# A new head, natural logits by transposes, increments behind the gathering, and an early softmax of c, in a fused attention and expert kernel

## Chip, cores, metric

The kernel runs on one core of one Trainium2 chip. The metric is the device time of one execution in microseconds (us), the median of three runs. The engines are TensorE (PE, with its weight loads as PEld), VectorE (DVE), ScalarE (ACT), GpSimd (POOL) and SyncE (SP), which here only issues DMAs.

## The reference

```python
# 1: linear attention with decay; batch 4, 8 heads, 768 steps, head size 48
for t in range(S):
    cur = einsum('bhd,bhe->bhde', u[None] * kt, vt)
    y[:, :, t] = einsum('bhd,bhde->bhe', rt, state + cur)
    state = wt[:, :, :, None] * state + einsum('bhd,bhe->bhde', kt, vt)
# 2: gated MLP on x = y as 3072 x 384; w_in 384 x 2048, w_out 2048 x 384
h = x @ w_in;  x = (h * clip(h + 3, 0, 6) / 6) @ w_out
# 3: soft mixture of 8 experts with 4 slots each, hidden size 1024
logits = x @ phi                                   # 3072 x 32
d = softmax of logits over the tokens;  slot_input = d.T @ x
slot_out[e] = max(slot_input[e] @ w1[e], 0) @ w2[e]
c = softmax of logits over the slots;   out = c @ slot_out
```

## The kernel before

The 3072 tokens are 24 tiles ("units") of 128, in six groups of four: tile n is sequence part n // 4 of batch n % 4. Every engine has its program written out by hand, and semaphores order them.

**Head.** `for n in range(B)` treats the first four tiles. TensorE does for each: `score` (8 heads as pairs in two row halves, 16 passes, L421), `turn_keys` (L430), `diagonal` of the next tile (8 passes of 2 columns, L458), `attend_first` (16 passes of 48 columns, L471), `increment` (L446), `turn_x` (L500) and one `stay_warm` (a 512-column matmul of no use but to keep the engine working, L532). VectorE scans the decays of the next tile (`scan_suffix` L773, `restart_prefix` L778, `scan_prefix` L785), masks the scores (`mask_first` L809), finishes y (L818), multiplies r by its decays (L794) and takes the low half of x (`low_x`, L833). GpSimd multiplies keys by decays (`decay_keys`, L1256) and r by k (`multiply_rows`, L1234), ScalarE copies out of PSUM. SP's queue sends the rows of four tiles, half of w_in, the rows of tile 4, w_outT, and, as buffers come free, the rows of tile 5 and the other half of w_in.

**Steps.** Then a loop over s runs 96 steps (16 per group of four tiles). Step s makes one block of 128 hidden units for the 512 tokens of group s // 16: `mlp(s)`, nine matmuls of 512 columns (three K-tiles, each as high*high, high*low, low*high in 16-bit halves, L514 to L516), into one of two PSUM banks; ScalarE makes the relu (L1123), VectorE gates (L860) and transposes (`turn_gated`, L870). mlp(s) waits for the gate of s - 2. Between them stands attention for the coming group's tiles, one tile per four steps by phase: score in phase 0, mask (L799) and scan in 1, keys, increment in 2, `attend` (L483 to L493) and prefix scan in 3. `low_scores` on GpSimd (L1247) makes the low half of the scores after ScalarE's high half (L1082).

**w_in's halves.** The weights are split into 16-bit halves in eight pieces: `high_w` on ScalarE (L1111), `low_w` on VectorE (L850), piece s // 2 + 1 in each even step of group 0.

**Group ends.** phi is folded into w_out beforehand (`weigh_phi`, L524). `add_logits` (L544) sums logits in four row blocks; ScalarE copies them to `l_part`, `fold_logits` (L551) sums the blocks. In step 2 of the next group VectorE finds the maximum, ScalarE makes alpha (the rescaling of earlier groups) and then `weight` = exp (L1138); VectorE transposes it (L892). `natural_logits` (L556) makes logits with tokens in rows, in step 2; ScalarE copies them (`copy_logits`, L1142). In step 3 follow the increment and `gather_slots`, 64 small matmuls in four banks (L570), which VectorE adds to `acc` in step 4.

**Tail.** After the last gathering the banks are copied out (L1193 on ScalarE, L1030 on VectorE), folded with the inverse sum, transposed, multiplied by w_out, and given to the experts: `apply_w1` (L686), transposes, `apply_w2` (L711), `pick_slots` (L720), the final matmuls (L754) and 12 stores. The softmax of c over all 24 tiles is made in the same stretch (VectorE L1025 to L1046, ScalarE L1190 and L1198), and `turn_c` (L704), three times eight transposes of c, stands between the expert matmuls.

## Time and profile before

| | |
|---|---|
| runs | 452.33, 452.84, 454.29 us; median 452.84 |
| profiled execution | 455.68 us; its span, from the first to the last instruction, 454.0 |
| mean granted TensorE clock | 0.946 |
| busy share of the span | PE 94%, PEld 52%, DVE 75%, ACT 33%, POOL 40% |
| DMA | 69.35 MB, 153 GB/s over the span |

"x16" behind a row says that it stands for sixteen instructions. A row's duration of a matmul holds the time in which it overlaps the next one, so what a pass costs is read from the distance of two starts. The granted clock is the share of TensorE's full clock: 1.00 is 2.4 GHz, 0.50 is 1.2 GHz.

### The profile page before, as it was taken

Reading aid. Unit: us, or ns where it says so; the run is one execution under the profiler, and the core shown is the slowest. Engines: PE = TensorE matmul, PEld = TensorE weight load, DVE = VectorE, ACT = ScalarE, POOL = GpSimd, SP = SyncE. Lnnn points to the kernel's source line nnn. Section 1 sums busy time; section 2 is a strip of 40 time slices with the busy share of each in tenths; the row PEclk is TensorE's granted clock in tenths of the full one; section 3 lists DMA queues with packets and bytes.
Section 4 is the critical chain, followed back from the end, with each engine's and each line's share of the span. In section 5 each row is a group of like instructions: output and inputs, shape, how many; then the busy total and the mean of one; then the engine's idle time right before and its main releaser. Section 6 shows DMA issues by size and latency. Waiting matters only on the chain.

```text
span 454.0 us, 9636 instructions
## 1 busy us (share of the span) xinstructions
PE 427.3 (94%) x3891; PEld 238.2 (52%) x3891; DVE 340.9 (75%) x539; ACT 148.4 (33%) x250; POOL 180.1 (40%) x174
## 2 busy tenths in 40 slices
PE   7999997888999999999999999998999999999982
PEld 3898654444555555556555555464554534433420
DVE  7555589989998989888898998889776676472233
ACT  1221323542433334414344144342432323212122
POOL 5614255575544565446556435654370000000000
PEclk9555699999999999999999999999999999999987
DMA  8996130341933222340343213330005963469919
GB/s 215 300 381 223 61 115 1 115 113 64 337 107 114 77 70 83 115 116 11 104 116 113 86 31 114 114 114 18 37 2 206 423 222 124 181 250 423 395 62 359
DMA packets 15245, 69.35 MB, mean 153 GB/s; under 512 B 2016, under 2 KB 2656, under 8 KB 13152
## 3 DMA queue, kind: packets, MB, share of 16 engines
q1 hardware_dynamic: 15200, 68.73, 43.7%
q8 instruction: 31, 0.51, 0.4%
q14 instruction: 14, 0.11, 0.1%
HBM read 64.00 MB, written 4.72 MB: 151 GB/s over the span
## 4 chain that ended last, share of the span: by engine, by line
issue 39%; PE 33%; POOL 19%; DVE 4%; DMA 1%; ACT 1%; POOLq 0%; SPq 0%; DVEq 0%
POOL att L1256 5%; PE hid L514 4%; PE hid L516 4%; PE hid L515 4%; POOL att L1228 4%; POOL att L1226 3%; POOL att L1241 3%; POOL att L1274 3%; PE hid L711 2%; PE l_ps L570 2%; PE l_ps L544 2%; PE y_ps L471 2%; PE sc_ps L421 1%; PE hid L686 1%; PE sc_ps L686 1%
## 5 line engine op out<-in xcount | busy, mean ns | idle before, releaser
L1123 ACT ACTIVATE relu<-hid,three 128x512 f32<-128x512 f32 x96 | 65.9, 687 | 149.6 <-PE hid L516 149.0
L514 PE MATMUL hid<-x_split,w_split 128*128 128x512 f16 x288 | 109.9, 381 | 3.5 <-DVE gated L860 3.5
L515 PE MATMUL hid<-x_split,w_split 128*128 128x512 f16 x288 | 109.6, 380 | 0.0
L516 PE MATMUL hid<-x_split,w_split 128*128 128x512 f16 x288 | 109.4, 380 | 0.0
L860 DVE SCALAR_TENSOR_TENSOR gated<-relu,hid 128x512 f32<-128x512 f32 x96 | 65.2, 680 | 29.6 <-ACT relu L1123 29.0
L870 DVE STREAM_TRANSPOSE ring<-gated 128x512 f32<-128x512 f32 x96 | 68.3, 711 | 3.3
L1247 POOL TENSOR_TENSOR att<-att 128x1024 f16<-128x1024 f32 x20 | 39.9, 1996 | 64.6 <-ACT att L1082 64.6
L1265 POOL TENSOR_TENSOR att<-att 112x512 f32<-112x512 f32 x19 | 24.3, 1280 | 68.7 <-DVE att L785 68.7
L514 PEld LDWEIGHTS hid<-x_split,w_split 128*128 128x128 f16 x288 | 28.3, 98 | 40.8 <-issue 9.6
L516 PEld LDWEIGHTS hid<-x_split,w_split 128*128 128x128 f16 x288 | 28.2, 98 | 34.4 <-issue 0.5
L515 PEld LDWEIGHTS hid<-x_split,w_split 128*128 128x128 f16 x288 | 28.2, 98 | 25.2 <-issue 0.6
L1256 POOL TENSOR_TENSOR att<-att 112x512 f32<-112x512 f32 x22 | 29.6, 1343 | 14.4 <-DVE att L773 10.3
L421 PEld LDWEIGHTS sc_ps<-att 48*128 48x128 f32 x384 | 26.7, 210 | 16.2 <-issue 14.5
L421 PE MATMUL sc_ps<-att 48*128 48x128 f32 x384 | 31.6, 309 | 3.3 <-issue 2.1
L483 PE MATMUL y_ps<-att 112*128 112x96 f32 x160 | 33.7, 295 | 0.6 <-DVE att L844 0.3
L818 DVE SCALAR_TENSOR_TENSOR att<-y_ps,att 128x384 f32<-128x384 f32 x24 | 13.2, 549 | 24.2 <-PE y_ps L471 13.2
L773 DVE TENSOR_TENSOR_SCAN att<-att 112x517 f32<-112x517 f32 x22 | 28.0, 1272 | 1.3 <-POOL att L1256 1.1
L785 DVE TENSOR_TENSOR_SCAN att<-att 112x517 f32<-112x517 f32 x22 | 27.8, 1265 | 0.1
L483 PEld LDWEIGHTS y_ps<-att 112*128 112x128 f32 x160 | 25.0, 189 | 5.6 <-issue 3.7
L570 PE MATMUL l_ps<-ring,soft 32*32 32x512 f32 x192 | 25.5, 594 | 2.0 <-DVE soft L892 2.0
L570 PE MATMUL sc_ps<-ring,soft 32*32 32x512 f32 x384 | 26.1, 598 | 0.0
L1105 ACT ACTIVATE x_split<-y_ps 128x384 f16<-128x384 f32 x24 | 11.8, 490 | 43.2 <-PE y_ps L500 42.7
(202 smaller groups left out, 768.7 us busy)
## 6 DMA issues: line engine op xcount, KB each, us to landing
att<-nat_dram SPq DMA_DIRECT2D x20, 576.0 KB, 4.2
att<-rkT_dram SPq DMA_DIRECT2D x22, 448.0 KB, 5.6
att<-w_dram SPq DMA_DIRECT2D x5, 1536.0 KB, 14.1
att<-wT_dram SPq DMA_DIRECT2D x22, 226.2 KB, 4.7
out_dram<-w_split SPq DMA_DIRECT2D x12, 384.0 KB, 3.9
stage<-w_in_dram SPq DMA_DIRECT2D x2, 1536.0 KB, 13.7
ring<-w_outT_dram SPq DMA_DIRECT2D x1, 3072.0 KB, 17.2
stage<-w_dram SPq DMA_DIRECT2D x2, 1536.0 KB, 9.2
```

The lines of the kernel that those rows point to most:

```text
L421: last = pe.matmul(sc_bank[j][:, cols], k_dec[n % 2][rows, cols], r_dec[n % 2][rows, cols], start=True, stop=True)
L483: pe.matmul(both, r_dec[n % 2][0:PD, p * P:(p + 1) * P], state[b][0:PD, p, :], start=True, stop=False, skip_group_check=True)
L514: pe.matmul(hid[s % 2][:], high, x_high, start=(q == 0), stop=False)
L515: pe.matmul(hid[s % 2][:], high, x_low, start=False, stop=False)
L516: last = pe.matmul(hid[s % 2][:], low, x_high, start=False, stop=(q == KT - 1))
L570: ins = pe.matmul(dg_bank[a][SLOTS * c:SLOTS * (c + 1), :], weight_T[SLOTS * a:SLOTS * (a + 1), b * SLOTS:(b + 1) * SLOTS], ring_group(g, ...
L773: nc.vector.tensor_tensor_scan(suffix[0:PD, ::-1], w_rows_of(n)[0:PD, ::-1], mark[0:PD, ::-1], 1.0, ALU.mult, ALU.add).then_inc(suffix_don ...
L860: nc.vector.scalar_tensor_tensor(gated_tile(s), relu_tile(s), 6.0 * GATE, hid[s % 2][:], ALU.min, ALU.mult).then_inc(gated_done, 1)
L870: nc.vector.transpose(ring_tile(s), gated_tile(s)).then_inc(gated_turned, 1)
L1123: nc.scalar.activation(relu_tile(s), hid[s % 2][:], ACT.Relu, bias=three[:], scale=GATE / H_SCALE)\
L1247: nc.gpsimd.tensor_tensor(scores_lo, scores, scores_hi, ALU.subtract).then_inc(scores_lo_done, 1)
L1256: nc.gpsimd.tensor_tensor(dst, keys, decay, ALU.mult).then_inc(k_dec_done, 1)
```

## The change

In the head the idle matmuls are cut in three parts that wait for the scans, and two more stand ahead of each `attend_first` and one behind the diagonal; the diagonal's matmuls write their two columns 48 times, attend_first computes two heads' columns at once (the second is overwritten by its own matmul); the diagonal goes behind attend_first, the increment behind turn_x; GpSimd clears the state first; the fold matrix is made by ScalarE. Around step 0 the increment of tile 4, the third weigh_phi and sum_diag move back, the gates of steps 0 and 1 and the scan of tile 5 forward. Low halves 2 to 7 of w_in are made by GpSimd, from pieces that ScalarE scales first. At group ends the weight is made ahead of alpha; the first 32 rows of the folded logits are copied to SBUF, and natural_logits becomes transposes of these, just ahead of gather_slots (behind it in the last group), with the increment behind it. The softmax of c for 20 of 24 tiles is made in the last group (GpSimd, VectorE, ScalarE), in place; turn_c(0) and (1) go ahead of the last gathering; the first pick_slots goes behind the last apply_w2, and half of w2[4] is loaded earlier, into x_late. Buffers that stood there move. The core of the diff:

```diff
-        def split_at(s):
-            return s // 2 + 1 if s % 2 == 0 and s // 2 + 1 < W_PIECES else None
+        def scaled_behind(s):
+            return {0: 3, 4: 4, 5: 5, 8: 6, 9: 7}.get(s)
+
+        def split_behind(s):
+            return {1: 2, 2: 3, 5: 4, 6: 5, 9: 6, 10: 7}.get(s)
...
                 load_nat(n)
-            sp.wait_ge(w_lo_done, W_PIECES)
+            sp.wait_ge(w_lo_done, 2)
+            sp.wait_ge(w_lo_rest_done, W_PIECES - 2)
             for e in range(2):
...
                 sp.dma_start(w1_place[e], w1[e]).then_inc(w1_in[1], 16)
+            sp.dma_start(x_late, w2[4][:, 0:UNIT // 2]).then_inc(w2_late_in[0], 16)
             sp.wait_ge(l_ready, STEPS)
...
                 cols = slice(half * UNIT // 2, (half + 1) * UNIT // 2)
-                for e in (4, 6, 7):
+                for e in (6, 7) if half == 0 else (4, 6, 7):
                     sp.dma_start(w2_place[e][:, cols], w2[e][:, cols]).then_inc(w2_late_in[half], 16)
...
                 for p in range(PB):
-                    last = pe.matmul(hid[1][:, 2 * p:2 * p + 2], rk_prod[n % 2][0:PD, p * P:(p + 1) * P],
-                                     u_rows[0:PD, 2 * p:2 * p + 2], start=True, stop=True, skip_group_check=True)
+                    last = pe.matmul(hid[1][:, p * 2 * D:(p + 1) * 2 * D].rearrange("p (o j) -> p o j", j=2),
+                                     rk_prod[n % 2][0:PD, p * P:(p + 1) * P],
+                                     u_rows[0:PD, 2 * p:2 * p + 2].rearrange("p (o j) -> p o j", o=1)
+                                     .broadcast_to([PD, D, 2]), start=True, stop=True, skip_group_check=True)
                 last.then_inc(diag_ready, 1)
...
                     for j in range(2):
-                        cols = slice((2 * p + j) * D, (2 * p + j + 1) * D)
+                        h = 2 * p + j
+                        cols = slice(h * D, min(h + 2, H) * D)
                         last = pe.matmul(y_ps[:, cols], scores[:, (j * PB + p) * P:(j * PB + p + 1) * P],
...
             def natural_logits(g, n):
+                pe.wait_ge(l_copied, g + 1)
                 pe.wait_ge(state_added, min(n, LAST_INC) - B)
                 for t in range(B):
-                    last = pe.matmul(inc_ps[:, DM + t * SLOTS:DM + (t + 1) * SLOTS], l_part[:, t * P:(t + 1) * P],
-                                     fold32, start=True, stop=True, skip_group_check=True)
+                    last = pe.transpose(inc_ps[:, DM + t * SLOTS:DM + (t + 1) * SLOTS],
+                                        l_part[0:SLOTS, t * P:(t + 1) * P], ident[0:SLOTS, 0:SLOTS])
                 last.then_inc(nat_logits_ready, 1)
...
                 pe.wait_ge(weight_turned, g + 1)
+                pe.wait_ge(l_copied, g + 1)
                 for r in range(4):
...
             pe.wait_ge(warm_zeroed, 1)
-            for _ in range(16):
-                pe.matmul(hid[0][:, :], warm[:, 0:P], warm[:, P:P + GT], start=True, stop=True, skip_group_check=True)
+            keep_awake(10)
+            pe.wait_ge(suffix_done, 1)
+            keep_awake(4)
+            pe.wait_ge(prefix_done, 1)
+            keep_awake(3)
             score(0, None)
+            turn_keys(0)
             pe.wait_ge(pool_consts, 2)
             pe.wait_ge(ident16_done, 1)
+            stay_warm(2, hid[0])
             diagonal(0)
...
                     score(n, None)
-                turn_keys(n)
+                    turn_keys(n)
+                stay_warm(2, hid[0])
+                attend_first(n)
                 if n + 1 < B:
                     diagonal(n + 1)
-                else:
-                    stay_warm(2, hid[0])
-                attend_first(n)
+                stay_warm(1, hid[0])
+                turn_x(n)
                 increment(n, None)
-                turn_x(n)
                 stay_warm(1, hid[0])
...
                     weigh_phi(0)
+                if s == 1:
                     increment(B, s)
...
                     pe.wait_ge(x_lo_done, UNITS)
-                    stay_warm(6, y_ps)
+                    pe.wait_ge(c_lo_done, 1)
+                    pe.wait_ge(c_hi_done, 2)
+                    turn_c(1)
+                    pe.wait_ge(gated_done, STEPS - 1)
+                    stay_warm(3, hid[0])
                 if s == STEPS + 1:
-                    stay_warm(3, y_ps)
+                    turn_c(0)
                 if s == STEPS + 3:
-                    stay_warm(9, y_ps)
+                    stay_warm(9, hid[0])
                 if g >= 1 and i == 1:
...
                         weigh_phi(1)
-                        weigh_phi(2)
                     if is_unit(n):
...
                         turn_x(B)
-                    if g >= 1 and i == 2:
-                        natural_logits(g - 1, n)
                 if phase == 2:
+                    if g >= 1 and i == 3:
+                        if g < C:
+                            natural_logits(g - 1, n)
+                        gather_slots(g - 1, n)
+                        if g == C:
+                            natural_logits(g - 1, n)
                     if n < LAST_INC:
                         increment(n, s)
-                    if g >= 1 and i == 3:
-                        gather_slots(g - 1, n)
                 if phase == 3:
...
                         add_logits(g - 1, 3)
+                if s == 2:
+                    weigh_phi(2)
...
+            pe.wait_ge(c_hi_done, 4)
             turn_c(2)
...
                 pe.wait_ge(q, 2)
-            pe.wait_ge(cT_done, 1)
             pe.wait_ge(w2_early_in, 32)
...
             apply_w2(1, 0)
-            pick_slots(0)
             pe.wait_ge(w2_late_in[1], 48)
             apply_w2(1, 1)
-            pick_slots(EG - 1)
+            for g in range(EG):
+                pick_slots(g)
             pe.wait_ge(stack_hi_done, 1)
...
+                ins.then_inc(chain, 1)
+                dve.wait_ge(chain, chained[0])
+
+            def c_inverse(part):
+                cols, tiles = c_parts[part]
+                dve.wait_ge(c_exp_done, part + 1)
+                then(nc.vector.tensor_reduce(csum[:, tiles], by_slot(soft[:, cols]), AX_X, ALU.add))
+                then(nc.vector.tensor_scalar(csum[:, tiles], csum[:, tiles], 1e-9, None, ALU.add))
+                then(nc.vector.reciprocal(csum[:, tiles], csum[:, tiles]))
+                nc.vector.tensor_scalar(csum[:, tiles], csum[:, tiles], SOFT_SCALE, None, ALU.mult).then_inc(c_inv_done, 1)
+
+            def copy_cT(n):
+                dve.wait_ge(c_turned[n], 1)
+                nc.vector.tensor_copy(cT[n][0:3 * SLOTS].rearrange("p (b o) n -> p o b n", o=2),
...
+                if n == 2:
+                    low_w(0)
             low_x(B - 1)
-            low_w(0)
+            scan_suffix(B + 1)
+            restart_prefix(B + 1)
             mask_first(B)
             low_v(B)
-            sum_diag(B)
...
                 g, i = divmod(s, FT)
+                if s <= 1:
+                    gate(s)
+                    turn_gated(s)
                 if phase == 0:
...
+                    sum_diag(B)
                 if phase == 3:
...
                         add_slots(g - 1)
-                if s == 3:
+                if s == 4:
                     dve.wait_ge(w_phi_ready, 4)
                     nc.vector.transpose(w_phi[:], l_ps[:]).then_inc(w_phi_done, 1)
-                c = split_at(s)
-                if c is not None and c >= 2:
-                    low_w(c)
-                if 0 < s < STEPS:
+                if s == STEPS - 12:
+                    cols, tiles = c_parts[0]
+                    dve.wait_ge(logits_done, C - 1)
+                    nc.vector.tensor_reduce(cmax[:, tiles], by_slot(soft[:, cols]), AX_X, ALU.max).then_inc(c_max_done, 1)
+                if s == STEPS - 8:
+                    c_inverse(0)
+                if s == STEPS:
+                    copy_cT(1)
+                    copy_cT(0)
+                if 1 < s < STEPS:
                     gate(s)
...
-            chained = [0]
-
-            def then(ins):
-                chained[0] += 1
-                ins.then_inc(chain, 1)
-                dve.wait_ge(chain, chained[0])
-
-            def by_slot(ap):
-                return ap.rearrange("p (i s) -> p i s", s=SLOTS)
...
                 .then_inc(slots_done, 1)
-            dve.wait_ge(c_hi_done, 2)
-            nc.vector.scalar_tensor_tensor(c_split[:, :, 1, :], by_slot(soft), SOFT_SCALE, c_split[:, :, 0, :],
-                                           ALU.mult, ALU.subtract).then_inc(c_lo_done, 1)
+            dve.wait_ge(c_hi_done, 4)
...
+            def scale_w(c):
+                act.wait_ge(w_hi_done, c + 1)
+                nc.scalar.activation(stage[:, c * WP:(c + 1) * WP], stage[:, c * WP:(c + 1) * WP], ACT.Copy,
+                                     scale=W_IN_SCALE).then_inc(w_scaled, 1)
+
             def copy_diag(n):
...
                 if g:
+                    act.wait_ge(run_sum_done, g)
+                nc.scalar.activation(weight, l_ps[:], ACT.Exp, bias=neg_max).then_inc(weight_done, 1)
+                act.wait_ge(folded, g + 1)
+                nc.scalar.activation(l_part[0:SLOTS, :], l_ps[0:SLOTS, :], ACT.Copy).then_inc(l_copied, 1)
+                if g:
                     act.wait_ge(acc_added, 4 * g)
                     nc.scalar.activation(alpha, run_max[1 - g % 2], ACT.Exp, bias=neg_max).then_inc(alpha_done, 1)
-                    act.wait_ge(run_sum_done, g)
-                nc.scalar.activation(weight, l_ps[:], ACT.Exp, bias=neg_max).then_inc(weight_done, 1)
...
+            def c_exp(part):
+                cols = c_parts[part][0]
+                act.wait_ge(c_sub_done, part + 1)
+                nc.scalar.activation(soft[:, cols], soft[:, cols], ACT.Exp).then_inc(c_exp_done, 1)
+
+            def c_high(part):
+                cols, tiles = c_parts[part]
+                act.wait_ge(c_norm_done, part + 1)
+                for a in (0, 2):
+                    nc.scalar.activation(c_split[:, tiles, a, :], by_slot(soft[:, cols]), ACT.Copy).then_inc(c_hi_done, 1)
+
             act.wait_ge(pool_consts, 2)
             nc.scalar.activation(ident16_sb[:], ident[:], ACT.Copy).then_inc(ident16_done, 1)
+            make_fold()
             copy_diag(0)
...
                     copy_diag(n + 1)
+                high_x(n)
                 first_state(n)
-                high_x(n)
-                if n < 2:
-                    high_w(n)
+                if n == 1:
+                    high_w(0)
+                    high_w(1)
+                if n == 2:
+                    high_w(2)
+                    scale_w(2)
             high_v(B)
...
                         copy_keys(n)
-                c = split_at(s)
-                if c is not None and c >= 2:
-                    high_w(c)
                 if s < STEPS:
...
                     copy_keys(B)
+                c = scaled_behind(s)
+                if c is not None:
+                    high_w(c)
+                    scale_w(c)
                 if g >= 1 and i == 2:
                     weigh(g - 1)
+                if g >= 1 and i == 3:
                     copy_logits(g - 1)
-
-            def by_slot(ap):
-                return ap.rearrange("p (i s) -> p i s", s=SLOTS)
-
-            act.wait_ge(c_sub_done, 1)
-            nc.scalar.activation(soft, soft, ACT.Exp).then_inc(c_exp_done, 1)
+                if s == STEPS - 10:
+                    c_exp(0)
+                if s == STEPS - 5:
+                    c_high(0)
+
+            c_exp(1)
             for a in (0, 2):
...
+            def low_w(c):
+                pool.wait_ge(w_scaled, c - 1)
+                per = FT // W_PIECES
+                nc.gpsimd.tensor_tensor(w16[:, c * per:(c + 1) * per, 1].rearrange("p i q m -> p i (q m)"),
+                                        stage[:, c * WP:(c + 1) * WP].rearrange("p (i n) -> p i n", i=per),
+                                        w16[:, c * per:(c + 1) * per, 0].rearrange("p i q m -> p i (q m)"),
+                                        ALU.subtract).then_inc(w_lo_rest_done, 1)
+
             def diag_values(n):
...
-            decay_keys(0)
-            multiply_rows(0)
             for b in range(B):
...
             last.then_inc(state_zeroed, 1)
-            multiply_rows(1)
+            decay_keys(0)
+            pool.wait_ge(r_dec_done, 1)
+            multiply_rows(0)
             for n in range(B):
                 decay_keys(n + 1)
+                if n + 1 < B:
+                    multiply_rows(n + 1)
                 diag_values(n)
-                if n + 2 < B:
-                    multiply_rows(n + 2)
             decay_state(B)
+            decay_keys(B + 1)
             diag_products(B)
...
             diag_values(B)
-            decay_keys(B + 1)
...
                         decay_state(n + 1)
-
+                c = split_behind(s)
+                if c is not None:
+                    low_w(c)
+
+            cols, tiles = c_parts[0]
+            pool.wait_ge(c_max_done, 1)
+            nc.gpsimd.tensor_tensor(by_slot(soft[:, cols]), by_slot(soft[:, cols]), per_tile(cmax[:, tiles]), ALU.subtract)\
+                .then_inc(c_sub_done, 1)
             nc.gpsimd.memset(slot_inT, 0.0).then_inc(slots_zeroed, 1)
-            pool.wait_ge(hid_ready, STEPS)
-            pool.wait_ge(gated_done, STEPS)
+            pool.wait_ge(c_inv_done, 1)
+            nc.gpsimd.tensor_tensor(by_slot(soft[:, cols]), by_slot(soft[:, cols]), per_tile(csum[:, tiles]), ALU.mult)\
+                .then_inc(c_norm_done, 1)
+            pool.wait_ge(c_hi_done, 1)
+            nc.gpsimd.tensor_tensor(c_split[:, tiles, 1, :], by_slot(soft[:, cols]), c_split[:, tiles, 0, :],
```

## Rows read from the trace of the kernel before

**Rows 1.** The page's slices: TensorE's granted clock in tenths, 40 equal slices of 11.35 us.

```profile
PEclk9555699999999999999999999999999999999987
```

**Rows 2.** Stages: from:to us, their length, then each engine's busy us, clock, DMA.

```profile
9.30:12.70 3.40, 2.13 (x20) 1.80 (x16) 3.37 (x5) 0.72 (x2) 3.40 (x7) 0.97 1.12 276
...
12.70:53.70 41.00, 41.00 (x251) 34.99 (x251) 21.82 (x33) 9.49 (x22) 14.18 (x13) 0.50 0.77 257
...
51.34:75.00 23.66, 21.06 (x195) 11.88 (x194) 19.85 (x28) 8.86 (x14) 11.74 (x9) 0.95 0.19 61
...
67.90:71.00 3.10, 1.03 (x18) 0.54 (x16) 2.79 (x3) 2.56 (x5) 3.10 (x2) 1.00 0.00 0
...
75.00:121.70 46.70, 41.41 (x359) 22.68 (x355) 43.31 (x61) 17.39 (x27) 27.39 (x22) 1.00 0.41 143
...
121.70:181.00 59.30, 59.30 (x606) 34.08 (x603) 51.74 (x86) 22.60 (x37) 33.17 (x31) 1.00 0.30 94
...
436.00:439.40 3.40, 1.34 (x9) 0.52 (x6) 1.20 (x3) 0.97 (x2) 0.00 (x0) 0.97 0.00 0
```

**Rows 3.** Timeline of TensorE, head, second tile: start us, us, engine, line, operation.

```profile
19.47 2.08 PE L421 MATMUL sc_ps<-att 48*128 48x128 f32 x16
...
23.88 3.63 PE L471 MATMUL y_ps<-att 128*128 128x48 f32 x16
...
27.44 1.09 PE L446 MATMUL inc_ps<-att 128*64 128x48 f32 x16
...
29.72 2.08 PE L421 MATMUL sc_ps<-att 48*128 48x128 f32 x16
```

**Rows 4.** Timeline of TensorE at full clock: first scores, first diagonal, a 96-column pair.

```profile
8.29 1.16 PE L421 MATMUL sc_ps<-att 48*128 48x128 f32 x16 [1.20 <-POOL att L1256]
...
9.72 1.02 PE L458 MATMUL hid<-spare,att 112*128 112x2 f32 x8 [0.27 <-POOL att L1234]
...
59.15 0.44 PE L483 MATMUL y_ps<-att 112*128 112x96 f32 x2
```

**Rows 5.** Timeline of VectorE in the head: a scan beside GpSimd, one alone, a mask.

```profile
8.34 2.22 DVE L773 TENSOR_TENSOR_SCAN att<-att 112x517 f32<-112x517 f32 x1 [1.14 <-POOL att L1256]
...
28.62 1.23 DVE L773 TENSOR_TENSOR_SCAN att<-relu,att 112x517 f32<-112x517 f32 x1
...
31.87 1.29 DVE L809 TENSOR_TENSOR att<-sc_ps,mask 128x512 f32<-128x512 f32 x2 [1.36 <-PE sc_ps L421]
```

**Rows 6.** DMA issues from 18 to 21 us: size, us from issue to landing.

```profile
att<-rkT_dram SPq DMA_DIRECT2D x1, 448.0 KB, 18.7
...
att<-wT_dram SPq DMA_DIRECT2D x1, 226.2 KB, 17.6
```

**Rows 7.** Waits from 60 to 121 us: us in total, times, longest.

```profile
POOL att L1247 <- ACT att L1082: 8.9, 4, 2.4
...
PE hid L514 <- DVE gated L860: 3.5, 3, 1.2
...
PE inc_ps L446 <- ACT att L1099: 2.0, 3, 0.9
```

**Rows 8.** Two lines' instructions: ns min/median/max, first and last start.

```profile
L850 DVE SCALAR_TENSOR_TENSOR w_split<-stage,w_split x8: 923/940/2124, 50.0 to 107.3; 128x768 f16<-128x768 f32 x8
...
L1247 POOL TENSOR_TENSOR att<-att x20: 1993/1996/1999, 53.9 to 335.9; 128x1024 f16<-128x1024 f32 x20
```

**Rows 9.** Timeline at the end of group 1: the weights and their transpose.

```profile
189.24 0.67 ACT L1138 ACTIVATE soft<-l_ps,stats 128x512 f32<-128x512 f32 x1
...
190.28 0.67 DVE L892 STREAM_TRANSPOSE soft<-soft 128x512 f32<-128x512 f32 x1
```

**Rows 10.** Timeline of the tail: last bank copies, second pick.

```profile
402.89 0.59 ACT L1193 ACTIVATE soft<-sc_ps 128x512 f32<-128x512 f32 x1
...
403.18 0.68 DVE L1030 COPY spare<-k_ps 128x512 f32<-128x512 f32 x1
...
436.81 0.86 PE L720 MATMUL k_ps<-att,relu 128*96 128x384 f32 x2 [0.78 <-ACT att L1207]
```

119 lines of the change are left out of this document (69 added, 50 removed).

## Prediction

> **What bounds the kernel now.** I read the page's slices first [rows 1]: TensorE is busy nearly everywhere, but its granted clock stands near half in slices 2 to 5 and is full behind them. The stage table [rows 2] says the same in microseconds: from 12.7 to 53.7 TensorE is busy 41.00 of 41.00 us at a granted clock of 0.50, the 1.2 GHz level. So the head (attention of the first four tiles, up to the first expert step at 51.34) is bound by a TensorE that never waits and runs at half speed. Then comes group 0 of the gated MLP: 23.66 us for its first five steps, and TensorE busy 41.41 of 46.70 us up to the end of the group. Group 1 has 59.30 of 59.30: from there TensorE's own work is the bound, and nothing is won but by taking work from it or from the tail, where softmax, gathering and expert layers hang on each other.
>
> **The head.** At half clock one tile takes 10.25 us, from one score's start to the next (19.47 to 29.72) [rows 3]: scores, key turns and diagonal up to 23.88, attention to 27.44, the rest 2.28. The change gives each tile three more 512-column matmuls, widens the 8 diagonal passes from 2 to 96 columns and the 16 attention passes from 48 to 96. That is more work, 24 wider passes, and pays only if the clock stays full. Does it? The clock fell at 12.7 behind a stretch with TensorE busy 2.13 of 3.40 us, mostly two-column and key passes, and at 439.4 behind 1.34 of 3.40; it did not fall over 67.9 to 71.0, where PE was busy 1.03 of 3.10 [rows 2], the increment passes and the ends of expert matmuls. It never rose in the head, busy as that was with narrow passes. These rows don't say what would have kept it; but in the new head each narrow stretch has 512-column matmuls before and behind it and is itself twice as wide or more, so it is nearer to the two stretches that held or were left alone (67.9 to 71.0, the expert steps) than to the two that fell. I take it that the clock holds. The Trainium skill, "TensorE: Matmul & The Clock Gate", Part 1, says that a busy engine gets its full clock; by that alone the old head would have had it and the widening would be worth nothing, and the trace (41.00 us busy, 0.50) disagrees.
>
> One tile at full clock: scores 1.1 [rows 4] plus key turns 0.5; attention 16 passes at 0.14 = 2.25 (the 96-column passes of later tiles [rows 4]: pairs start 0.43 apart, at 59.15 and 59.58, with six short passes of 0.15 together between them); diagonal 8 x 0.14 = 1.13; half of the 2.28 for increment, turn of x and one idle matmul = 1.14; three more 512-column matmuls at 0.22 = 0.65. Sum 6.8 us. The VectorE chain beside it, from one attention's end to the next one's first mask half: finish y 0.56, decay 0.68, suffix scan 1.23, reciprocal 0.18, low x 0.53, half a mask 0.65 [rows 5] (scan and mask; the others are single VectorE instructions of the same tile), with hand-overs some 4.2, against 6.8 less 2.25 = 4.5 on TensorE. It is hidden by 0.3. The first scores can't start before 8.3 [rows 4] (key DMA and decay, unchanged). From there: scores and turns 1.6, four idle matmuls 0.9, diagonal 1.1, attention 2.25: first attention ends at 14.1. Three more tiles 20.4, a VectorE low half of w_in between them 0.6 late, then y, turn, increment, scores of tile 4 together 3.0: first expert step at 38.1 against 51.34, **-13.2 us**. Bounds: passes that cost as at 2 columns (1.02 us for 8, about 0.11 each [rows 4]) give 35; scans slowed as the one that ran beside GpSimd (2.22 for 1.23 [rows 5]) cost 0.65 per tile, and the rows of tile 5, which landed at 36.9 and 38.4 [rows 6] and which now stand ahead of tile 4's mask on VectorE, can hold it too: 41. The DMA engines were full up to 41, so these landings move little.
>
> **Group 0.** First five steps: TensorE's own work is five steps at 1.95 (9.75), three weigh_phi at 0.97, two attentions at 1.8, score 1.1, turns and increments 2.3: 19.7 of 23.66. The new order puts the gates first, the increment and the third weigh_phi a step later; but VectorE's prefix scan for tile 5 and the GpSimd decay behind it still release the scores late, as does low_scores for the first attention. I take 21.1: **-2.5**; bounds -0.7 (only the first step's half clock) and -3.9. The rest of the group idles 5.3 us (46.70 less 41.41), and the waits say why [rows 7]: VectorE's gates and low halves, ScalarE's copies. Six low halves (0.94 us each, once 2.12 beside GpSimd [rows 8]) leave VectorE. They go to GpSimd at 768/1024 of its 2.00 us subtraction, 1.5 each, 9.0 in ten steps where it stood idle a third of the time; the two a tile lie in its waits for ScalarE's high scores (8.9 us over four [rows 7]). ScalarE gets six scalings of 0.83, beside relus only. Gain **-4.0**, bounds 0 (contention gives it all back) and -5.3. The Trainium skill, "GPSIMD Engine Reference", 3.1, speaks against this edit: 2.6 cycles per element for two inputs, VectorE twice as fast. By its figure, an estimate, a low half takes 1.7 instead of 1.5 us, 1 us more in all, on an engine that waits.
>
> **Group ends.** Eight natural-logit passes (0.97) become four transposes (about 0.5), and the increment goes behind the gathering: TensorE has 0.4 less. But what releases the gathering is the chain weight (ends 189.91), its transpose on VectorE (190.28 to 190.95) [rows 9]. That engine comes to the transpose only then, whatever ScalarE does, so the gathering moves from 191.2 to 191.0 and has 0.5 of increment behind it: +0.3 in two groups, 0 in the others, where the new 0.6 us copy of the logits plus 0.5 of transposes end with the transpose. **+0.5**, bounds -2 (TensorE's saving kept) and +2.
>
> **Last group.** Softmax of c for 20 of 24 tiles moves here: on VectorE a reduction of 0.8 and later 1.6 us of sum and inverse, on ScalarE an exp and two copies of 0.7, on GpSimd three idle-time operations. VectorE has 0.5 us to spare a step; **+0.5**, bounds 0 and 2.
>
> **Tail.** Weight before alpha: -0.2. Natural logits behind the gathering: ScalarE's copy of them, VectorE's maximum and subtraction, and the exp now stand between the gathering's end and the copies of its banks, which before were ready (ScalarE ended 403.48, VectorE 403.86 [rows 10], gathering 402.5). 0.7 of transposes, 0.3 copy, 0.6 maximum and subtraction, 0.3 exp, 1.2 for two copies: 3.1 behind the gathering against 1.4, less some overlap, +1.2. Sixteen turns of c (0.5 for eight) leave the expert chain: -1.0; they now stand where idle matmuls stood. The first pick (0.9) goes behind the last expert matmul, where TensorE waited 0.78 us for ScalarE [rows 10]: -0.9. Sum **-1.0**, bounds -2.5 and +1. The w2 loads, one half earlier, end with their use or before.
>
> **Sum.** -13.2 -2.5 -4.0 +0.5 +0.5 -1.0 = -19.7. The profiled execution took 455.7 (span 454.0): 436.0, span 434.3. The median of three runs is 452.84, 2.8 lower, so **433**.
>
> **Rivals.** 1: the clock falls in the first tile as before, and does not rise. Then each tile is 10.25 plus 1.3 for three idle matmuls plus 24 passes each between 0.03 and 0.06 longer, 12.2 to 13 less 1 for what overlaps, so 11.6 to 12.6, and the first expert step starts at 54.7 to 57.7, 3.4 to 6.4 late. With the wide passes at twice the full-clock price (6.4) and half of group 0's gain (3.2) the time is 456, slower; it is slower from where the head loses more than group 0 gives. For it: no narrow stretch was ever seen to hold the clock over a whole tile. Against: 67.9 to 71.0. At the lower price it is 450 to 452, no change. 2: it falls in a later tile: each tile at half costs 5 more, 438 to 449. 3: GpSimd becomes the bound of group 0 (its low halves delay decay_keys, then the scores): group 0 gains nothing and the landings hold the head to 41: 433 + 6.5 + 3 = 442. 4: the edits at group ends and tail work as TensorE's savings suggest, and the head at its lower bound: 426.
>
> **How the numbers follow.** Forecast 0.70 (426 to 439). Rival 1 0.10, half of it slower and half no change. Rival 2 0.07, rival 3 0.08, rival 4's low end 0.05. The range 424 to 443 leaves out rival 1 and most of rival 2. 0.5% (2.3 us) is about what this measurement can tell from no change: faster 0.88, same 0.06, slower 0.06.
>
> **What would show it.** Granted clock 1.0 from about 6 us to 53; 6.8 us from score to score in the head; first expert step near 38; TensorE idle under 2 us in the last 11 steps of group 0; gatherings no earlier against the step before; final bank copies near 3 us behind the last gathering; no turn of c but eight in the expert chain. I am wrong if the clock row shows 0.5 in the head, or if tile 5's landings or the GpSimd subtractions appear as releasers.

## The result, and the profile after

| | before | after |
|---|---|---|
| runs | 452.33, 452.6, 452.84, 454.29 | 435.09, 438.5, 438.78, 438.99 |
| median | 452.72 | 438.64 |
| profiled execution, span | 455.68, 454.0 | 438.5, 436.8 |
| mean granted clock of the profiled execution | 0.946 | 0.983 |

The ratio of the mean times is 0.9665, with a 95% interval of 0.961 to 0.972 (the medians alone give 0.969): the changed kernel is 14 us faster. 433 was predicted.

To see where the time went, I cut both profiled executions at the starts of expert steps, the first matmul of `mlp(s)`. All numbers are us.

| stretch | before | after | difference | predicted |
|---|---|---|---|---|
| head: to step 0 | 51.35 | 37.67 | -13.7 | -13.2 |
| steps 0 to 5 | 23.65 | 21.28 | -2.4 | -2.5 |
| 5 to 16, rest of group 0 | 41.84 | 37.17 | -4.7 | -4.0 |
| group ends: 16-20, 32-36, 48-52, 64-68 | 19.46, 20.03, 20.03, 20.47 | 19.78, 20.67, 22.18, 21.73 | +4.4 | +0.5 |
| 80 to 95, last group | 39.95 | 39.92 | 0.0 | +0.5 |
| from step 95 to the end | 65.40 | 64.60 | -0.8 | -1.0 |
| span | 453.97 | 436.79 | -17.2 | -19.7 |

The steps between the group ends are equal within 0.02 in both. The last group's row holds its own group end, 15.27 and 15.22.

The granted clock of the changed kernel, in the page's 40 slices of 10.9 us. The low digits at the start [rows 1] are gone, and an 8 has come twice in the middle:

```profile
PEclk9999999999999999999998999989999999999996
```

The windows of the changed kernel, with the columns of [rows 2]: the head from 12.70 on, the first five steps, the rest of group 0, and the piece of a group end that makes the first of those 8s.

```profile
12.70:37.67 24.97, 23.93 (x251) 18.85 (x249) 20.16 (x30) 10.54 (x23) 13.92 (x11) 1.00 1.02 370
37.67:58.95 21.28, 20.21 (x195) 11.40 (x194) 18.13 (x26) 9.39 (x15) 18.42 (x13) 1.00 0.33 96
58.95:96.12 37.17, 36.09 (x311) 19.85 (x307) 34.71 (x52) 19.72 (x30) 30.06 (x24) 1.00 0.40 130
230.60:234.00 3.40, 3.31 (x64) 1.26 (x65) 3.33 (x8) 0.41 (x2) 0.00 (x0) 0.50 0.02 5
```

The head runs at 1.00 where it ran at 0.50 [rows 2]. In the rest of group 0 TensorE's idle time is 1.1 us (37.17 less 36.09), where it was 5.3. The last row shows the new loss: TensorE is busy, at half clock.

One tile of the new head, timeline of TensorE. The next score starts 6.60 us behind this one (10.25 in [rows 3]); the 16 wide attention passes take 1.80 up to the diagonal, 0.112 each, and the diagonal 0.93 up to the next idle matmul:

```profile
23.40 1.16 PE L446 MATMUL sc_ps<-att 48*128 48x128 f32 x16
...
25.47 1.96 PE L499 MATMUL y_ps<-acc,att 128*128 128x96 f32 x16
27.27 1.10 PE L483 MATMUL hid<-spare,att 112*128 112x96 f32 x8
...
30.00 1.16 PE L446 MATMUL sc_ps<-att 48*128 48x128 f32 x16
```

The end of group 1 in the changed kernel, three timelines. First VectorE: the maxima, the gate and turn of the step, then the turn of the weight (L941).

```profile
166.50 0.66 DVE L926 TENSOR_REDUCE stats<-l_ps 128x1 f32<-128x512 f32 x1
167.19 1.21 DVE L928 TENSOR_TENSOR stats<-stats 128x1 f32<-128x1 f32 x1
168.44 0.15 DVE L935 TENSOR_SCALAR stats<-stats 128x1 f32<-128x1 f32 x1
168.52 0.69 DVE L909 SCALAR_TENSOR_TENSOR gated<-relu,hid 128x512 f32<-128x512 f32 x1
169.24 0.71 DVE L919 STREAM_TRANSPOSE ring<-gated 128x512 f32<-128x512 f32 x1
169.87 0.67 DVE L941 STREAM_TRANSPOSE soft<-soft 128x512 f32<-128x512 f32 x1
```

Then TensorE: transposes of the logits, first gathering passes, and the increment behind them.

```profile
169.84 0.43 PE L593 MATMUL inc_ps<-ident,soft 32*128 32x32 f32 x4 [1.21 <-ACT soft L1204]
170.80 0.63 PE L614 MATMUL l_ps<-ring,soft 32*32 32x512 f32 x4 [0.53 <-DVE soft L941]
...
175.18 0.67 PE L471 MATMUL inc_ps<-att 128*64 128x48 f32 x16
```

The same place one group later, where the clock falls; a group of gathering passes now takes 1.08, not 0.63:

```profile
229.73 0.43 PE L593 MATMUL inc_ps<-ident,soft 32*128 32x32 f32 x4 [1.22 <-ACT soft L1204]
230.69 1.08 PE L614 MATMUL l_ps<-ring,soft 32*32 32x512 f32 x4 [0.53 <-DVE soft L941]
```

And again one group later, where the gathering starts at full clock and loses it 0.8 us in:

```profile
290.21 0.43 PE L593 MATMUL inc_ps<-ident,soft 32*128 32x32 f32 x4 [1.60 <-ACT soft L1204]
291.18 0.63 PE L614 MATMUL l_ps<-ring,soft 32*32 32x512 f32 x4 [0.53 <-DVE soft L941]
...
292.05 1.38 PE L614 MATMUL l_ps<-ring,soft 32*32 32x512 f32 x4
```

So ahead of the four gatherings TensorE stands idle 0.33, 1.21, 1.22 and 1.60 us in front of the transposes and each time another 0.53 behind them, and in two of the four the clock falls at the start of the gathering or within its first microsecond.

### The profile page after: what moved, and what is told of

Its sections match the earlier page's. It is cut to its first block, busy times and chain, and to the rows that moved or that the text cites. A ratio compares the mean times of both kernels' runs of the same rounds, so it can differ in the third digit from the quotient of the medians.

```text
span 436.8 us, 9636 instructions
## 1 busy us (share of the span) xinstructions
PE 410.5 (94%) x3874; PEld 219.7 (50%) x3874; DVE 334.2 (77%) x535; ACT 158.2 (36%) x269; POOL 195.7 (45%) x183
## 4 chain that ended last, share of the span: by engine, by line
PE 72%; DVE 9%; issue 7%; DMA 5%; POOL 4%; ACT 2%; SPq 0%; POOLq 0%; DVEq 0%
PE hid L545 12%; PE hid L547 12%; PE hid L546 12%; PE l_ps L580 5%; PE l_ps L614 5%; PE y_ps L511 5%; DMA att<-rkT_dram 4%; PE sc_ps L446 4%; PE hid L762 2%; PE inc_ps L471 2%; DVE gated L909 2%; PE y_ps L528 2%; DVE att L822 2%; PE sc_ps L614 1%; PE hid L743 1%
## 5 line engine op out<-in xcount | busy, mean ns | idle before, releaser
L1358 POOL TENSOR_TENSOR att<-att 112x512 f32<-112x512 f32 x19 | 22.5, 1182 | 58.7 <-DVE att L834 58.7
L614 PE MATMUL l_ps<-ring,soft 32*32 32x512 f32 x192 | 28.4, 664 | 3.5 <-DVE soft L941 2.9
L1349 POOL TENSOR_TENSOR att<-att 112x512 f32<-112x512 f32 x22 | 26.9, 1224 | 8.0 <-DVE att L822 6.5
L446 PEld LDWEIGHTS sc_ps<-att 48*128 48x128 f32 x384 | 23.3, 187 | 12.3 <-issue 12.3
L614 PE MATMUL sc_ps<-ring,soft 32*32 32x512 f32 x384 | 29.1, 664 | 0.0
L446 PE MATMUL sc_ps<-att 48*128 48x128 f32 x384 | 27.9, 284 | 1.1 <-issue 1.1
L614 PE MATMUL k_ps<-ring,soft 32*32 32x512 f32 x192 | 28.5, 663 | 0.0
```

The source lines that it names most:

```text
L446: last = pe.matmul(sc_bank[j][:, cols], k_dec[n % 2][rows, cols], r_dec[n % 2][rows, cols], start=True, stop=True)
L614: ins = pe.matmul(dg_bank[a][SLOTS * c:SLOTS * (c + 1), :], weight_T[SLOTS * a:SLOTS * (a + 1), b * SLOTS:(b + 1) * SLOTS], ring_group(g, ...
```

## The experiments

Two theories stood against each other. **A**: the group ends lose by their new order (natural logits and increment), partly through the clock. **B**: what is missing was lost elsewhere, in the tail or by GpSimd's new work. Each time is a median, and each ratio is of mean times, to the kernel before, run on the same chip beside it. The stages are those of one profiled execution of each kernel. "..." in an edit stands for lines left out. Kernels whose name begins with ue or um start from the changed kernel with undone group ends; the um ones, but for um_turns, also have the maximum of ue_max.

**fill**: idle matmuls into the two waits.

```diff
                         if g < C:
+                            if is_unit(n):
+                                pe.wait_ge(masked, 2 * n + 2)
+                            stay_warm(5, sc_bank[0])
                             natural_logits(g - 1, n)
+                            stay_warm(2, sc_bank[0])
                         gather_slots(g - 1, n)
```

> The changed kernel with seven 512-column matmuls of no use at each of the first five group ends: five ahead of the natural logits, two behind them, in a PSUM bank that is free there; all else as changed. Theory A: at a group end TensorE waits 1.2 us for the copied logits and 0.5 us for the turned weights, and the nearly idle stretch lets the clock fall in some gatherings (two of five in the profiled run), 1.5 us each; the fillers stand in the waits, so the clock stays full to the last stores, the four steps with a gathering take 20.7 us or less instead of 22.2 and 21.7, and the time is 435 to 436. Theory B: the group ends are longer because of the new order alone; the fillers change nothing but cost up to 0.2 us each: 438.6 or 439.

436.94 (436.59 to 437.06), ratio 0.963, 95% interval 0.959 to 0.966. The clock falls only in the tail. The group ends take 20.41, 20.67, 20.67, 20.24: the two long ones of after are gone, but 20.67 is still 0.64 above before. So the falls go when the waits are filled, and something else makes the 0.64. The idle matmuls are not free where the wait is short: the first group end takes 0.6 more than in after (20.41 for 19.78) and the last group's own 1.0 more (16.20 for 15.22), which is why 3.0 us of falls saved give only 1.7 in the median.

**undo_ends**: everything at group ends and behind the last gathering as before (order of natural logits, increment, alpha; eight passes for four transposes), head, group 0 and early softmax of c as changed.

```diff
-                    last = pe.transpose(inc_ps[:, DM + t * SLOTS:DM + (t + 1) * SLOTS],
-                                        l_part[0:SLOTS, t * P:(t + 1) * P], ident[0:SLOTS, 0:SLOTS])
+                    last = pe.matmul(inc_ps[:, DM + t * SLOTS:DM + (t + 1) * SLOTS], l_part[:, t * P:(t + 1) * P],
+                                     fold32, start=True, stop=True, skip_group_check=True)
...
+                    if g >= 1 and i == 2:
+                        natural_logits(g - 1, n)
                 if phase == 2:
-                    if g >= 1 and i == 3:
-                        if g < C:
-                            natural_logits(g - 1, n)
-                        gather_slots(g - 1, n)
-                        if g == C:
-                            natural_logits(g - 1, n)
                     if n < LAST_INC:
                         increment(n, s)
+                    if g >= 1 and i == 3:
+                        gather_slots(g - 1, n)
```

> The changed kernel with the edits at group ends undone: natural logits by matmuls a step earlier, the increment ahead of the gathering, alpha ahead of the weight, no copy of the folded logits. Theory A: both the falls of the clock (3 us in two gatherings) and the order's own cost (0.3 to 0.6 at four ends, 1.2 in the tail) go; four steps with a gathering take 20.0 as before the change, the tail is 1 us shorter; 438.6 - 4.3 - 1 = 433.3. Theory B (the order costs nothing but for the clock): 435.5. If the falls stem from something else in the change, such as the new head, they stay: 437.

432.11 (432.05 to 432.41), ratio 0.952 (0.949 to 0.955). Group ends 19.27, 20.03, 20.03, 20.12, and 63.43 from step 95 to the end, where after has 64.60. A holds: this part of the change costs 6.5 us of the medians (438.64 less 432.11, from two chips). Its place is seen in the timeline of TensorE at the end of group 1, to be read against the rows of after above:

```profile
169.24 0.67 PE L471 MATMUL inc_ps<-att 128*64 128x48 f32 x16 [0.69 <-ACT att L1147]
169.83 0.63 PE L612 MATMUL l_ps<-ring,soft 32*32 32x512 f32 x4
```

This group end starts (step 32) at 154.20, that of after at 155.12. So the gathering begins 15.63 us into it here and 15.68 in after: nearly the same, as VectorE's turn of the weight ends at the same place in both (169.63 here and 170.54 in after, 15.43 into the group end). Here the natural passes and the increment are done by then. In after the natural passes are shorter and the increment (0.6) still follows: TensorE's saving turned into waiting, and work that had filled the wait stands behind it.

**inc_first**: the increment ahead of the gathering again, the transposes behind it in all groups.

```diff
-                    if g >= 1 and i == 3:
-                        if g < C:
-                            natural_logits(g - 1, n)
-                        gather_slots(g - 1, n)
-                        if g == C:
-                            natural_logits(g - 1, n)
                     if n < LAST_INC:
                         increment(n, s)
+                    if g >= 1 and i == 3:
+                        gather_slots(g - 1, n)
+                        natural_logits(g - 1, n)
```

> The changed kernel with the increment ahead of the gathering (its wait for the copied natural logits of the same group taken to the group before) and the natural logits behind it at every group end, as it is in the last. Theory A: the increment's 0.6 us fills the wait for the weights, no wait for the copied logits stands ahead of the gathering; the clock stays full, four steps with a gathering take 19.6 (20.0 before the change, less 0.4 of shorter logits); 438.6 - 4.3 - 1.5 = 432.8 to 434. Theory B: half a microsecond won at most, 438.

436.06 (435.68 to 440.68), ratio 0.963 (0.959 to 0.967), with group ends 19.62, 20.68, 20.68, 20.60: a miss. The timelines of ScalarE and TensorE say why:

```profile
168.73 0.57 ACT L1201 ACTIVATE soft<-l_ps 32x512 f32<-32x512 f32 x1
169.21 0.28 ACT L1204 ACTIVATE stats<-stats 128x1 f32<-128x1 f32 x1
169.39 0.52 ACT L1148 ACTIVATE att<-k_ps 128x448 f32<-128x448 f32 x1
```
```profile
169.96 0.67 PE L471 MATMUL inc_ps<-att 128*64 128x48 f32 x16 [1.82 <-ACT att L1148]
```

The new copy of the logits stands in ScalarE's order ahead of the copy of the keys, for which the increment waits. The gathering begins 0.30 us later than in undo_ends (15.93 for 15.63 us into the group end), and the four transposes now stand behind it, the other 0.35. So putting the increment back alone leaves the order's cost. The clock stays up in the profiled execution, though TensorE's waits ahead of the gathering, 1.82, 1.82 and 2.57 us, are longer than those of after: the length of a wait alone does not decide it. One run of 440.68, 4.6 above the median, was not profiled.

**ue_max**: in undo_ends, one operation of one element a partition in another form.

```diff
-                    nc.vector.tensor_tensor(run_max[g % 2], run_max[1 - g % 2], group_max, ALU.max)\
+                    nc.vector.tensor_scalar(run_max[g % 2], group_max, run_max[1 - g % 2], None, ALU.max)\
...
```

> The same base; the running maximum is a VectorE tensor_scalar with the old maximum as its per-partition scalar, in place of a tensor_tensor with two SBUF inputs (1.21 us for one element in the trace, ended just behind a 2.0 us GpSimd subtraction; 0.16 where GpSimd stood idle). Theory A, the two-input form waits for GpSimd's instruction: it falls to 0.2 us, weights come 1 us earlier, the increment doesn't wait, the three group ends behind the first take 19.3 instead of 20.0 and 20.1, the time is 430. Theory B, the duration is not GpSimd's doing: still 1.2 us, 432.

429.64 (429.43 to 429.79), ratio 0.945 (0.943 to 0.946), 2.5 us less than undo_ends: **the fastest kernel here, 25.6 us below the kernel before beside it (455.19).** Group ends 19.28, 19.27, 19.27, 19.13. In VectorE's timeline the maximum took 0.21 us, and the operation behind it started 1.0 earlier against the group's start. TensorE's gathering gains 0.75 of that (14.88 for 15.63 us into the group end): then TensorE no longer waits ahead of it.

```profile
165.52 0.66 DVE L922 TENSOR_REDUCE stats<-l_ps 128x1 f32<-128x512 f32 x1
166.22 0.21 DVE L924 TENSOR_SCALAR stats<-stats 128x1 f32<-128x1 f32 x1
166.47 0.15 DVE L931 TENSOR_SCALAR stats<-stats 128x1 f32<-128x1 f32 x1
```

**after_max**: the same edit in the changed kernel itself.

> The changed kernel with one edit: the maximum of the group and the running one, one element a partition, as an operation with a scalar operand (0.21 us in the run of the undone group ends with the same edit, 1.21 without). Theory: at a group end all times hang on the negative maximum; it comes 1.0 us earlier, so TensorE's wait ahead of the transposes shrinks from 1.21 to 0.2 and the clock stays up at 230 and 292. Four group ends at 19.7 instead of 20.67 and no falls: 436.8 less 3.0 less 4.4 = 429.5 of span, a time near 431.5. Rival: the order of TensorE's passes, not the length of the wait, makes the clock fall: it still falls at one or two group ends and the time is 433 to 435.

432.46 (432.25 to 436.44), ratio 0.955 (0.949 to 0.962). Group ends 19.80, 19.67, 19.69, 19.26, TensorE's first wait 0.22 and 0.23 us where it was 1.21 and 1.22 (0.34 and 0.62 in the other two), no fall there. That is A's forecast of the stages, and 1 us more in the median than expected. The shortening of one wait by 1.0 us goes with no fall at any group end, without any change of order, so the order alone does not explain them. Nor does the wait alone, by inc_first: that the falls take the two together fits both runs, but each rests on one profiled execution. The profiled execution of this kernel is its longest, 436.44, for a reason outside the group ends, told below.

**um_turns**: in the changed kernel the same maximum, ScalarE's copy of the logits ahead of the weight, and TensorE's order transposes, increment, gathering.

```diff
+                act.wait_ge(group_max_done if g else run_max_done, g or 1)
+                nc.scalar.activation(l_part[0:SLOTS, :], l_ps[0:SLOTS, :], ACT.Copy).then_inc(l_copied, 1)
                 act.wait_ge(neg_max_done, g + 1)
...
+                        natural_logits(g - 1, n)
                     if n < LAST_INC:
                         increment(n, s)
+                    if g >= 1 and i == 3:
+                        gather_slots(g - 1, n)
...
```

> The changed kernel with that maximum and another order at group ends: ScalarE copies the folded logits as soon as VectorE has read them, ahead of the weight; TensorE makes the four transposes first, then the increment, then the gathering, in all groups. Theory: with the maximum early TensorE's own work bounds the group end, and now the saving of four transposes (0.43) for eight passes (0.84) counts: 19.27 less 0.4 = 18.9 at each of four group ends, some 1.5 us less than with the group ends undone and the same maximum (429.6), so 428.1. Rival: the gathering still waits for the transpose of the weight behind VectorE's gate, and the saving is idle: 429.4 to 430.

431.56 (431.43 to 431.71), ratio 0.951 (0.946 to 0.957): 1.9 slower than ue_max, and neither forecast. Group ends 19.94, 19.73, 19.75, 19.25. The timeline of TensorE at the end of group 1:

```profile
168.59 0.43 PE L593 MATMUL inc_ps<-ident,soft 32*128 32x32 f32 x4
169.93 0.64 PE L471 MATMUL inc_ps<-att 128*64 128x48 f32 x16 [0.91 <-ACT logits L1210]
```

The transposes wait for nothing now, but the increment writes the bank from which ScalarE copies the natural logits, and this copy (169.53 to 169.78) stands in ScalarE's order behind the keys and the relu. The wait has moved from one chain to another.

**ue_narrow**: in undo_ends, the diagonal's passes at 2 columns and the attention passes at 48 again; idle matmuls stay.

```diff
-                        cols = slice(h * D, min(h + 2, H) * D)
+                        cols = slice(h * D, (h + 1) * D)
...
```

> Base: the changed kernel with the group ends undone (432.1). Here the head's attention and diagonal passes are narrow again, 48 and 2 columns as before the change; the idle 512-column matmuls and the order stay new. Theory A, the widened passes hold the clock: the granted clock falls in the head as before the change, a tile takes 11 us or more, the first expert step starts near 50, the time is 444 or more. Theory B, the idle matmuls alone hold it: the clock stays full, 24 passes a tile are up to 0.03 us shorter, the first expert step starts at 36.5 to 37.3, the time is 431.5 to 432.

442.62 (437.43 to 442.98, three runs; a fourth, of 447.25, is not in the ratio), ratio 0.970 (0.963 to 0.976). In the profiled execution the first expert step starts at 47.83. The window of the fall:

```profile
13.80:41.10 27.30, 27.30 (x170) 22.97 (x171) 14.62 (x22) 7.18 (x17) 8.50 (x9) 0.50 0.89 319
```

The clock fell at 13.8, in the first tile, and rose at 41.1, in the fourth. The widening is worth 10.5 us in the medians. The three times lie 5.5 us apart, at mean clocks of 0.961 and 0.972, so the fall does not seem to last equally long in each; one was profiled. The width itself cost nothing: the fourth tile's 16 narrow passes, at full clock again, took 1.96 us, as the wide ones of after.

**um_narrow_diag**: in ue_max, only the diagonal at 2 columns.

```diff
-                    last = pe.matmul(hid[1][:, p * 2 * D:(p + 1) * 2 * D].rearrange("p (o j) -> p o j", j=2),
...
+                    last = pe.matmul(hid[1][:, p * 2 * D:p * 2 * D + 2], rk_prod[n % 2][0:PD, p * P:(p + 1) * P],
...
```

> The kernel with undone group ends and the scalar maximum (429.6), with the diagonal's eight passes at 2 columns again and the attention passes left at 96. If the attention passes alone hold the clock, the head is as fast or 0.2 faster, 429.4; if both widenings are needed, the clock falls in the head for up to 27 us and the first expert step comes at 43 to 48: 435 to 440.

429.77 (429.67 to 429.92), ratio 0.947 (0.943 to 0.952), first expert step at 37.27, no fall in the head. Beside the idle matmuls, which stayed, the wide attention passes suffice; the wide diagonal neither costs nor gives.

**ue_no_idle**: in undo_ends, without the three idle matmuls ahead of and behind `attend_first` and the two ahead of the first diagonal.

```diff
-                stay_warm(2, hid[0])
                 attend_first(n)
                 if n + 1 < B:
                     diagonal(n + 1)
-                stay_warm(1, hid[0])
...
```

> The same base; the head keeps its wide passes but loses the idle 512-column matmuls around them (two ahead of the first diagonal, two ahead of each attention, one behind each diagonal); the one behind each increment stays, as before the change. Theory A, widened passes suffice: the clock stays full, TensorE does 0.65 us less for each tile, VectorE's chain of some 6.2 us then sets the tile, first expert step near 36, time 431. Theory B, the idle matmuls are needed: the clock falls and stays at half, first expert step at 48 to 52, time 443 to 447.

432.92 (432.23 to 434.56), ratio 0.952 (0.950 to 0.955). First expert step at 37.25, as in undo_ends, at full clock: with wide passes the idle matmuls are not needed. In the profiled execution steps 0 to 5 took 2.2 us more, but by a landing, in VectorE's timeline of the prefetched tile:

```profile
37.85 1.24 DVE L815 TENSOR_TENSOR_SCAN att<-att 112x517 f32<-112x517 f32 x1 [1.42 <-DMA att<-wT_dram]
```

In undo_ends this scan started at 36.35 and waited for nothing. The low scores on GpSimd followed it, 43.26 for 41.03, and with them the attention of tile 4, for which TensorE waited 2.0 us. Its other three runs took 432.23 to 432.96.

**ue_low_vec**: in undo_ends, low halves 2 to 7 of w_in on VectorE again, no scaled pieces.

```diff
-                c = split_behind(s)
-                if c is not None:
-                    low_w(c)
```
(on GpSimd, and for it on VectorE:)
```diff
+                c = split_at(s)
+                if c is not None and c >= 2:
+                    low_w(c)
```

> The same base; low halves 2 to 7 of w_in are made by VectorE again, in each even step of group 0 and with no scaling on ScalarE; GpSimd makes none. Theory A, VectorE bound group 0: steps 5 to 16 take 41.8 again instead of 37.2, steps 0 to 5 up to 1 us more than 21.3, the time is 437 to 438. Theory B, the order of the gates and the full clock brought most of it: steps 5 to 16 take 38 to 39, the time is 433 to 434.

439.06 (439.01 to 439.19), ratio 0.965 (0.964 to 0.967), 6.95 more than undo_ends: steps 0 to 5 22.64 for 21.28, 5 to 16 42.55 for 37.18. Moving them gave the whole gain of the rest of group 0, and more than half of that of the first steps. The edit also puts ScalarE's high halves back ahead of the relus, and the two were not tried apart. The waits of this run from 60 to 102 us speak for VectorE: TensorE waited 2.3 us for gates and its weight loads 2.5 for low halves, both on VectorE, and neither wait is in undo_ends; 1.7 went to ScalarE's copies of keys.

**um_pick**: in ue_max, the first pick again between the halves of the last expert matmul.

```diff
             apply_w2(1, 0)
+            pick_slots(0)
             pe.wait_ge(w2_late_in[1], 48)
```

> The kernel with undone group ends and the scalar maximum (429.6), with the first pick of slots ahead of the second half of the last expert matmul, as before the change. By the prediction's term the move behind it saved 0.9 us: 430.5 here. Rival: the pick filled a time in which TensorE waits anyway, or its move only shifted the wait: 429.6, no difference.

430.57 (430.5 to 430.82), ratio 0.949 (0.945 to 0.954): 0.93 more than ue_max, the predicted 0.9; in the profiled executions the stretch from step 95 to the end is 0.90 longer.

## Why the prediction was right, and which terms were off

**The head**, -13.7 for -13.2. The clock held. The prediction had said that its rows didn't tell what would keep it, and took it as likely for two reasons; one is shown, the wider attention passes (ue_narrow, um_narrow_diag), the other, the idle matmuls around them, is not borne out (ue_no_idle). A tile took 6.6 for 6.8: 16 attention passes at 0.112, not 0.14, are 0.45 less; VectorE, said to be hidden by 0.3, held TensorE twice (0.43 and 0.44 us in the fourth tile). Rival 1 did not come, but ue_narrow has its fall: 27.30 of 27.30 us busy at 0.50, until the clock rose in the fourth tile. By the Trainium skill, "TensorE: Matmul & The Clock Gate", Part 1, activity releases the throttle; that TensorE, busy throughout by the profile, stayed at the 1.2 GHz level for 27.30 us here and 41.00 in [rows 2] disagrees. Rival 1's sum has a slip: 12.2 to 13 less 1 is 11.2 to 12, not 11.6 to 12.6, so by its own terms its first expert step comes 1.6 to 2.4 us earlier than it says and its time is lower by as much. In ue_narrow a tile at half clock took 11.36 (its scores start at 17.52 and 28.88). In after_max and ue_no_idle the landing of tile 5 held VectorE's scan, one of the prediction's signs of being wrong; it did not in after.

**Group 0**, -2.4 for -2.5 and -4.7 for -4.0. The six low halves on GpSimd (L1325) took 1.80 us in the mean, not 1.5: five took 1.63 to 1.65, and one, beside a scan of VectorE, 2.58. They cost nothing. By the Trainium skill, "GPSIMD Engine Reference", 3.1, the estimate was 1.7, nearer than that from [rows 8]. Rival 3 did not come: the edit that it spoke against is worth 6.95 us.

**Group ends**, +4.4 for +0.5: this is the term that was mis-sized, and nearly all of what the terms missed (2.5 us in sum; this term is 3.9 off, the others together came 1.4 better than said). The step said that the gathering is released by VectorE's turn of the weight, "whatever ScalarE does", and has "0.5 of increment behind it". Both are in the trace. But it then counted "+0.3 in two groups, 0 in the others". Without the falls (after's first two group ends, fill's last two) the four differ from before by +0.32, +0.64, +0.64 and -0.23, 1.4 in sum. The starts of the gathering account for each: 14.80, 15.69, 15.69 and 15.85 us into the group end, where before had 15.07, 15.64, 15.63 and 16.08, and behind the first three stands the increment, about 0.6. So in the middle two the gathering came 0.05 later and not 0.2 earlier as forecast (in both kernels the turn of the weight ends 15.43 us in), with 0.6 behind it, and the first, not 0, had the increment behind it too. And with the waits that TensorE's saving and the new order left, 1.22 and 1.60 us ahead of the transposes and 0.53 behind them, the clock fell at two gatherings, 1.5 us each (22.18 less 20.67, 21.73 less 20.24), 3.0 in sum. The prediction had weighed the clock in the head alone, though it had read at 439.4 what a stretch with a TensorE mostly idle does.

**Last group and tail**, 0 for +0.5 and -0.8 for -1.0. The last group cost nothing in undo_ends either, where the early softmax of c stays (39.97 for 39.95), so that its work fits into VectorE's spare time whole. undo_ends takes back the natural logits behind the last gathering (+1.2 predicted) and the weight ahead of alpha (-0.2) together: 64.60 less 63.43, 1.2 for 1.0. The last bank copy ends 2.7 us behind the gathering (388.61 less 385.90), near the 3.1 of the prediction; um_pick the pick's -0.9. What is left, 65.40 to 63.43 less 0.9, is -1.0, as predicted for the turns of c. That last split is a remainder, not a run of its own.

**From the profiled execution to the median.** The prediction took 2.8 us off, since before's median was so much below its profiled execution. For the changed kernel they are equal (438.64 and 438.5), so this step made the forecast another 2.9 too low, as much as all the terms. Before's executions beside fill went from 450.69 (mean clock 0.96) to 455.84 (0.945) on one chip. Most of its time at half clock lies in its head, so the step took off a piece of a spread that the changed kernel no longer has; where exactly before's executions differ was not seen, only one was profiled. The changed kernel has a spread of its own: its run of 435.09 has a mean clock of 0.994 and is 3.4 us shorter than the profiled one at 0.983, about the price of the two falls. That it had none is an inference: it was not profiled, and in fill the mean clock goes from 0.985 to 0.994 while the time stays within 0.5 us.

**What stays open.** In the profiled execution of after_max the clock fell elsewhere, behind the attention of tile 4, which had waited 1.72 us for GpSimd's low scores:

```profile
47.30:54.10 6.80, 6.39 (x31) 2.81 (x32) 5.10 (x8) 0.00 (x0) 6.46 (x6) 0.50 0.61 190
```

Steps 0 to 5 took 25.44 for 21.3. Its three other runs (432.25 to 432.48) are 4 us shorter. The low scores were late for the same reason as in ue_no_idle, a landing, as VectorE's timeline shows:

```profile
38.08 1.24 DVE L822 TENSOR_TENSOR_SCAN att<-att 112x517 f32<-112x517 f32 x1 [1.51 <-DMA att<-wT_dram]
```

The load took 20.8 us to land, where after's took 16.2; why is open. In ue_no_idle the same wait, 2.0 us for the low scores, came with no fall, so what decides between the two is open too. So is why the clock fell at two group ends of after and not at the one with the same 1.21 us, nor in inc_first. Also not tried: the early softmax of c undone by itself, and ScalarE's copy of the natural logits moved ahead of the relu in um_turns.

## What to carry to other kernels

When work is taken from an engine ahead of a wait that another engine's chain ends, read the chain first: the saved time becomes idle, and independent work that filled the wait must not be moved behind it. Then look for an instruction in that chain that takes long for its size; here one element a partition took 1.21 us, and its other form gave 2.5 us (ue_max), while the reordering had cost 6.5. A clock that fell with narrow passes in one place and after short waits in another is a thing to price at every place where a wait grows, not only where it fell before.

## What the hardware showed that was not expected

- A VectorE maximum of two one-element operands took 1.20 to 1.21 us and ended 0.01 to 0.02 behind GpSimd's subtraction at the three group ends where this ran; at the other two maxima GpSimd stood idle and they took 0.16. From the first of the three, and the last:

```profile
166.40 1.99 POOL L1340 TENSOR_TENSOR att<-att 128x1024 f16<-128x1024 f32 x1 [3.24 <-ACT att L1134]
...
379.60 0.16 DVE L928 TENSOR_TENSOR stats<-stats 128x1 f32<-128x1 f32 x1
```

 The subtraction ended at 168.39, the maximum at 168.40. With one operand as a scalar it took 0.21 beside the same subtraction. The Trainium skill, "SBUF — State Buffer", "Who interferes with whom", says that a VectorE instruction with two SBUF inputs contends with a GpSimd one that reads SBUF. The trace agrees: the one-element maximum lasted until the subtraction was over.
- The same kernel with narrow passes in the head had runs from 437.43 to 442.98, with mean clocks of 0.972 and 0.961; with wide ones from 432.05 to 432.41. The wide passes took no longer than the narrow ones at full clock (16 in 1.96 us).
- A wait of 1.2 us ahead of the gathering was followed by a fall of the clock in one group and not in another of the same execution; with a wait of 0.2 us in its place there was none at any group end. With waits of 1.8 and 2.6 us in another order (inc_first) there was none either.
